# Attention queries stored column by column in eight interleaved blocks, and a dense prefetch that begins four passes later

## What is computed

```python
# attention: batch 2, heads 8, seq 768, head_dim 64, 8 memory rows, chunks of 32
for c in range(nc):
    q_c = q[:, :, c_start:c_end]
    k_full = np.concatenate([mem_k, k[:, :, l_start:r_end]], axis=2)
    v_full = np.concatenate([mem_v, v[:, :, l_start:r_end]], axis=2)
    scores = scale * np.matmul(q_c, k_full.transpose(0, 1, 3, 2))
    a = np.exp(scores - np.max(scores, axis=-1, keepdims=True))
    a = a / (np.sum(a, axis=-1, keepdims=True) + 1e-09)
    out[:, :, c_start:c_end] = np.matmul(a, v_full)
# dense: 1536 tokens, 512 -> 2048 -> 512
h = x @ w_in
y = (h * (1.0 / (1.0 + np.exp(-1.702 * h)))) @ w_out
# then: one of 8 experts per token, 512 -> 1024 -> 512, times its gate
```

## Time and profile before

| | us |
|---|---|
| median of 3 runs | 571.86 |
| lowest and highest | 567.55, 575.18 |
| the profiled execution, its own time | 572.34 |
| its span, first to last instruction | 570.6 |
| attention: first score matmul to end of the last values | 7.7 to 82.9 |
| mean granted TensorE clock | 0.97 of 2.4 GHz |

### The profile page before, as it was taken

The page is one execution under the profiler, slowest core; times in us unless marked ns, Lnnn a source line. Parts: engine busy times, 40 slices in busy tenths (PEclk is TensorE's granted clock), DMA queues, the critical chain, the costliest instruction groups (busy, mean ns, idle before and its releaser), DMA issues.

```text
span 570.6 us, 8633 instructions
## 1 busy us (share of the span) xinstructions
PE 534.4 (94%) x3228; PEld 453.2 (79%) x3228; DVE 286.4 (50%) x541; ACT 222.7 (39%) x374; POOL 174.8 (31%) x207
## 2 busy tenths in 40 slices
PE   7988889999999999999999999789999989999792
PEld 7878778888888878888887887679989878788582
DVE  4985666444233342213445545515445467756950
ACT  1443474334232221213334344114546366755520
POOL 2764530000000002000000300202576488999642
PEclk9996799999999999999999999898999999999997
DMA  7999919920000001001222532244947287766000
GB/s 206 254 267 242 213 48 350 286 68 0 1 0 2 1 1 71 4 0 38 74 75 75 181 114 75 93 130 150 337 141 278 83 312 248 263 237 223 22 24 30
DMA packets 33130, 74.39 MB, mean 130 GB/s; under 512 B 5423, under 2 KB 12335, under 8 KB 33072
## 3 DMA queue, kind: packets, MB, share of 16 engines
q1 hardware_dynamic: 28800, 66.97, 38.4%
q0 software_dynamic: 3840, 6.32, 3.1%
q10 hardware_dynamic: 432, 0.33, 0.2%
HBM read 60.97 MB, written 18.91 MB: 140 GB/s over the span
## 4 chain that ended last, share of the span: by engine, by line
PE 83%; DMA 5%; DVE 4%; issue 4%; POOL 1%; SPq 1%; ACT 1%; DVEq 0%; POOLq 0%
PE bank L1076 10%; PE bank L1078 10%; PE bank L1077 10%; PE bank L1120 8%; PE bank L1121 8%; PE bank L1122 8%; PE bank L1089 5%; DMA tile_in<-attention_tiles 5%; PE bank L1040 3%; PE bank L1293 3%; PE bank L1291 3%; PE bank L1292 3%; PE bank L1091 2%; PE bank L1191 2%; PE bank L1289 2%
## 5 line engine op out<-in xcount | busy, mean ns | idle before, releaser
L323 POOL TENSOR_TENSOR w_lo<-raw,w_hi 128x256 fp32r<-128x256 f32 x100 | 83.2, 867 | 51.8 <-ACT w_hi L307 51.7
L482 POOL DMA_INDIRECT dispatched_rows<-rows,slot_idx x12 | 11.9, 994 | 281.4 <-issue 147.8
L769 DVE SCALAR_TENSOR_TENSOR g<-g,bank 128x512 f32<-128x512 f32 x48 | 33.0, 688 | 112.6 <-ACT g L558 112.0
L307 ACT ACTIVATE w_hi<-raw 128x1024 fp32r<-128x1024 f32 x80 | 82.8, 1052 | 0.4 <-DMA raw<-expert_units 0.3
L558 ACT ACTIVATE g<-bank 128x512 f32<-128x512 f32 x48 | 28.8, 600 | 134.7 <-PE bank L1078 134.7
L323 DVE TENSOR_TENSOR w_lo<-raw,w_hi 128x1024 fp32r<-128x1024 f32 x55 | 75.4, 1371 | 8.3 <-ACT w_hi L307 8.0
L1120 PE MATMUL bank<-w_hi,g_hi 128*128 128x512 f32 x192 | 76.0, 396 | 1.5 <-issue 1.5
L1076 PE MATMUL bank<-x_hi,w_hi 128*128 128x512 f32 x192 | 76.7, 399 | 0.0
L1121 PE MATMUL bank<-w_lo,g_hi 128*128 128x512 f32 x192 | 75.8, 395 | 0.0
L1122 PE MATMUL bank<-w_hi,g_lo 128*128 128x512 f32 x192 | 75.8, 395 | 0.0
L1078 PE MATMUL bank<-x_hi,w_lo 128*128 128x512 f32 x192 | 75.7, 394 | 0.0
(11 more groups left out here) (119 smaller groups left out, 963.1 us busy)
## 6 DMA issues: line engine op xcount, KB each, us to landing
raw<-expert_units SPq DMA_DIRECT2D x64, 512.0 KB, 4.4
raw<-dense_units SPq DMA_DIRECT2D x16, 512.0 KB, 10.4
dispatched_rows<-empty SPq DMA_DIRECT2D x24, 257.0 KB, 12.6
slot_rows<-dispatched_rows SPq DMA_DIRECT2D x24, 257.0 KB
tile_in<-attention_tiles SPq DMA_DIRECT2D x12, 384.0 KB, 7.7
tile_in<-attention_tiles SPq DMA_DIRECT2D x12, 336.0 KB, 7.0
tile_in<-attention_tiles SPq DMA_DIRECT2D x12, 160.0 KB, 5.6
tile_in<-attention_tiles SPq DMA_DIRECT2D x12, 128.0 KB, 6.0
```

The costliest lines, as they stand in the source:

```text
L307: act.activation(w_hi[u % RING][:, :], raw[u % RING][:, :], ACT.Copy).then_inc(s_whi, 1)
L323: last = engine.tensor_tensor(w_lo[u % RING][:, part], raw[u % RING][:, part], w_hi[u % RING][:, part].bitcast(F32), ALU.subtract)
L769: dve.scalar_tensor_tensor(g32[i % 2][:, :], g32[i % 2][:, :], 1.0, h_bank[i % 2][:, :], ALU.add, ALU.mult).then_inc(s_g, 1)
```

## The change

Three things. First, the queries of a tile: the eight blocks are interleaved, so that column m of block x stands at column 8 m + x. The upper 64 partitions have their 64 x 8 query columns first and the zeros behind, the lower ones the reverse. A DMA row is now one run of 2048 bytes, the two query DMAs are 64 partitions by 512 columns each, together 256 KB where it was 288 KB, and the stationary matrix of block x is read with a stride of 8 columns, which is 32 bytes (`blocks[:, :, x]`). Second, both windows now have the same order of halves, so the values matmuls read the same side of the transposed probabilities in each. Third, `EARLY_FROM` is 9. The host lays the input out to match.

```diff
--- before.py
+++ after.py
@@ -42,10 +42,9 @@
     MAX_GROUPS = [GROUPS] + [[(0, NBL)]] * (B * S // P - 1)
     max_done = lambda t, g: sum(len(x) for x in MAX_GROUPS[:t]) + g + 1
     SCALE = 1.0 / D ** 0.5
-    Q_RUNS = 2 * NP + 1
-    QK = Q_RUNS * P + NP * SPAN
+    QK = NBL * P + NP * SPAN
     ATT = QK + WINDOWS * DM
-    Q_IN = (NP + 1) * P
+    Q_IN = NBL * HALF
     NSLOT = 3
     TB = 4
@@ -59,7 +58,7 @@
     UNITS = U0 + E * UE
     RING = U0
     EARLY = 8
-    EARLY_FROM = 5
+    EARLY_FROM = 9
     AHEAD = 4
     SLT = CAP // P
     SLOTS = E * CAP
@@ -291,14 +290,12 @@
             return (s_H, STEPS + EFT * e + 2 * r + 2) if r < UE // 2 else \
                 (s_Y, STEPS + EFT * e + 2 * (r - UE // 2) + 2)
-        def query_runs(n, half, odd):
-
-
-
-
-            runs = NP if odd else NP + 1
-            part = tile_in[n][half * D:(half + 1) * D, odd * P:odd * P + runs * 2 * P]
-            return part.rearrange("p (c x) -> p c x", x=2 * P)[:, :, 0:P]
+        def queries(n, half, place):
+
+
+
+
+            return tile_in[n][half * D:(half + 1) * D, place * Q_IN:(place + 1) * Q_IN]
         def split_hi(act, u):
             act.wait_ge(s_raw[u % RING], 16 * (u // RING + 1))
@@ -377,10 +374,9 @@
 
                 for half in range(2):
-                    there = attn_in[t, half * D:(half + 1) * D, 0:(NP + 1 - half) * P]
-                    sp.dma_start(query_runs(n, half, half), there.rearrange("p (c x) -> p c x", x=P))\
+                    sp.dma_start(queries(n, half, half), attn_in[t, half * D:(half + 1) * D, 0:Q_IN])\
                       .then_inc(s_qk[n], 16)
-                sp.dma_start(tile_in[n][:, Q_RUNS * P:QK], attn_in[t, :, Q_IN:Q_IN + NP * SPAN])\
+                sp.dma_start(tile_in[n][:, NBL * P:QK], attn_in[t, :, Q_IN:Q_IN + NP * SPAN])\
                   .then_inc(s_qk[n], 16)
             def load_values(t):
@@ -776,7 +772,7 @@
             for n in range(NSLOT):
                 for half in range(2):
-                    dve.memset(query_runs(n, half, 1 - half), 0.0).then_inc(s_zero_q, 1)
+                    dve.memset(queries(n, half, 1 - half), 0.0).then_inc(s_zero_q, 1)
             for t in range(-3, NT + 1):
                 if 0 <= t + 1 < NT - 1:
                     inverse(t + 1)
@@ -1035,10 +1031,11 @@
                 for g, (x0, x1) in enumerate(GROUPS):
                     if t >= 2:
                         pe.wait_ge(s_mask, NG * (t - 2) + g + 1)
+                    blocks = tile_in[n][:, 0:NBL * P].rearrange("p (m x) -> p m x", x=NBL)
                     for x in range(x0, x1):
-                        q0, k0 = HALF + x * P, Q_RUNS * P + x // WINDOWS * SPAN + x % WINDOWS * (HALF + M)
+                        k0 = NBL * P + x // WINDOWS * SPAN + x % WINDOWS * (HALF + M)
                         last = pe.matmul(score_bank[t % 2][g][:, (x - x0) * KEYS:(x - x0 + 1) * KEYS],
-                                         tile_in[n][:, q0:q0 + P], tile_in[n][:, k0:k0 + KEYS],
+                                         blocks[:, :, x], tile_in[n][:, k0:k0 + KEYS],
                                          start=True, stop=True)
                     last.then_inc(s_score, 1)
@@ -1063,8 +1060,7 @@
                         pe.wait_ge(s_pTa, NG * t + x // BPG + 1)
                     for half in range(2):
                         v0 = QK + w * DM + (2 * c + half) * D
-
-                        side = (half + w) % 2 * HALF
+                        side = half * HALF
                         last = pe.matmul(xT_bank[t % 2][half * D:(half + 1) * D, x * HALF:(x + 1) * HALF],
                                          tile_in[n][0:KEYS, v0:v0 + D],
                                          probT[t % 2][0:KEYS, x, side:side + HALF], start=True, stop=True)
@@ -1405,7 +1401,7 @@
     T, NT, TPB, KT = B * S, B * S // P, S // P, DM // P
     half = P // 2
     keys, span = half + LEFT + RIGHT + M, P + LEFT + RIGHT + 2 * M
-    q_in = (H // 2 + 1) * P
+    q_in = H * half
     f32 = np.float32
 
@@ -1413,8 +1409,9 @@
     for t in range(NT):
         b, s0 = t // TPB, t % TPB * P
         qt = q[b, :, s0:s0 + P].transpose(0, 2, 1)
-        attn[t, 0:D, half:half + H // 2 * P] = qt[0::2].transpose(1, 0, 2).reshape(D, -1)
-        attn[t, D:P, 0:H // 2 * P] = qt[1::2].transpose(1, 0, 2).reshape(D, -1)
+        for a in range(2):
+            blocks = qt[a::2].reshape(H // 2, D, 2, half).transpose(1, 3, 0, 2)
+            attn[t, a * D:(a + 1) * D, 0:q_in] = blocks.reshape(D, q_in)
         lo, hi = max(0, s0 - LEFT), min(S, s0 + P + RIGHT)
         kw = np.zeros((H, span, D), f32)
         vw = np.zeros((H, span, D), f32)
```

## The result

The changed kernel takes 584.02 us (median of 4 runs, 579.98 to 585.19) beside 572.09 for the one before (4 runs). The ratio is 1.020, with an interval of 1.012 to 1.029. So it is slower beyond the noise, though the interval does not tell whether by more than 2%. I had forecast 2.4% faster and a range of 553 to 579. The profiled execution takes 584.39 us, its span is 582.7.

What follows compares the result with a forecast made beforehand. Passes 3 to 8 were taken as bound by DMA, through the 512 KB unit in each turn. Terms -15.4 + 0.5 + 1.0 + 0.8 - 0.6 + 0 = -13.7 us from 572.34 gave 558.6, stated as 558.5; range 553 to 579.

Steps and rivals of the forecast that it cites:

- The strided weight load: Score matmuls' stationary loads with a stride of 8 words: taken as 0 us, at worst +1.86 us per tile if halved.
- Rival 1: The stride doubles the score load, TensorE bounds passes 0 to 8: +5.6 us, about 578; chance 0.21.
- start and first scores: Before pass 0: first three tiles' scores +4 us under the doubled load, earlier key issue -0.6 us.
- The prefetch: Passes 3 to 8, units moved four turns later: 23.1 us in place of 38.46, -15.4 us, no clock loss.
- rival 2: DMA stays the bound in part at 245 GB/s, passes 3 to 8 take 30.9 us: -7.5, near 565; chance 0.15.
- Does the DMA keep up?: Tile inputs in passes 3 to 8: 280 GB/s, 3.6 us per tile; 0 to +1.4 us, taken as +0.5.
- The two units in the way: Queries of tiles 10 and 11 behind one dense unit each: 0 to +4.7 us, taken as +1.0.
- The units in time: Dense units fetched later still land before ScalarE and the first dense steps want them: cost 0.
- the values: Values matmuls reading a different half of the tile in four of eight blocks: same count and shapes, 0.
- the tail: Pass 9, with VectorE and GpSimd late for pass 10 after a short pass 8: 4.35 us from 3.53, +0.8.
- Faster by over 2%: Chance that the whole time falls under 560.4 us: 0.50; slower by more, over 583.3, had 0.06.

Runs made afterwards that it cites:

- experiment 3: The changed kernel with the prefetch put back (EARLY_FROM = 5), so the strided load alone; 585.02 us, ratio 1.024 to the kernel before.
- experiment 5: The changed kernel with the stride for each tile's first four blocks only, neighbouring columns for the last four; 565.58 us, ratio 0.991 to the kernel before.
- experiment 2: The changed kernel with the stationary matrix read from neighbouring columns, its DMAs and prefetch kept; 560.49 us, ratio 0.980 to the kernel before.
- experiment 8: experiment 2 with one query DMA over 128 partitions in place of two of 64, same bytes; 552.11 us, ratio 0.972 to the kernel before.
- experiment 1: The kernel before with only the prefetch moved (EARLY_FROM = 9), neighbouring columns as before; 561.21 us, ratio 0.981.
- Experiment 7: The kernel before with the prefetch later still: EARLY_FROM = 11 took 556.95 us, ratio 0.975; EARLY_FROM = 10 took 558.12, ratio 0.977.

## Why the prediction was wrong

**The strided weight load** is the step that failed. I put the term at 0; it measured 2.0 us in each pass at the full clock (3.87 us for a tile's scores in place of 1.86), and 17.3 us by the start of pass 11, the lower clock included. I took 0 because an expert's rows show 128 neighbouring words read in 0.06 us, half of the 0.116 that the score load takes, and called this twofold slack. The slack is real for neighbouring words only. With each word on a line of its own 128 of them need 0.24 us, four times the 0.06, whatever the clock. So halving the best rate was the wrong reading of that row: the best rate is lost by a factor of four, as it would be if a read took one word where it could take four. The row is also of another kind of load: the expert's weights are rounded float32 (`fp32r`), the queries plain float32, and no run loads both with one stride. The Trainium skill (SBUF — State Buffer, Door 1: The DMA port swizzle) speaks of lines of 16 bytes and of two hits per line for the full rate; the runs agree, with 0.122 us at two words per line and 0.238 at one. With its lines the row would have given the right bound: 32 lines in 0.06 us are at most 1.9 ns each, 128 lines 0.24 us, an estimate. Its sentence that a stride of 4 fp32 is free the runs do not bear out.

**Rival 1** had the right mechanism, and put the time at 578 with a chance of 0.21. By its own terms: passes 0 to 2 +5.6 forecast, +6.7 measured; start and first scores +4.0 - 0.6 forecast, +2.7 measured, since the strided load hardly suffers from the low clock (48 first matmuls in 11.5 us, 0.240 each, where they took 8.3); passes 3 to 8 -4.2 forecast, +1.5 measured. The last is the gap, and most of it is the clock, which the rival left out. Six passes of 5.87 us would be 35.2, near its 34.3; they took 40.0. It was down in part of that stretch (mean 0.78) with TensorE never idle. In experiment 3 and with the stride of 16 bytes it was down in the same way (mean 0.75 from 27.2 to 81.5 us, and 0.82 from 27.5 to 80.6), again without idle time, while it held at 1.00 in experiment 5, where half of the loads are fast. My sentence that TensorE "never idles long, so I count no clock loss" took a row without idle time as enough for the full clock. That the waiting for weights is what lowers the clock is argued, not shown by a run that changes nothing else.

**The prefetch.** The step was right in kind and too large. Without the stride, in experiment 2, passes 3 to 8 take 60.68 - 29.67 = 31.0 us, -7.5 where my terms for them gave -15.4 + 0.5 + 1.0 = -13.9. That is rival 2 nearly to the number: it put them at 30.9 us, with 12.3 for passes 3 to 5 and 18.6 for 6 to 8, and 13.5 and 17.5 were measured. I gave it 0.15. So it is partly luck that experiment 2 ends at 560.5, near my 558.5: by the start of pass 11 only 6.3 of my 13.7 us are there, and the rest of the gain lies behind the logits, where I had said that nothing changes.

**Does the DMA keep up?** Mis-sized. I took 280 GB/s and 3.6 us per tile; it was 233 GB/s and 13.5 / 3 = 4.5 us in passes 3 to 5 of experiment 2, +0.65 per pass where my upper end was +0.23. I had put the rate down to the length of the rows; experiment 8 shows that the two query transfers of 64 partitions held it down.

**The two units in the way.** Forecast +1.0 of 0 to +4.7. In experiment 1 passes 7 and 8 take 62.17 - 48.30 = 13.9 us, 6.2 over two of 3.85: 2.5 us of wait, and most of the rest the low clock after it, which the term left out. Experiment 7 regains 4 us by moving the units. One count ahead of the prediction is wrong as well: with `EARLY_FROM` = 5 not four but six units have queries behind them (units 0 to 5, ahead of tiles 6 to 11). The sums don't use the four, since they take all of passes 3 to 8 as bound by the DMA.

**The units in time, the values, the tail** held in the changed kernel: no wait of ScalarE for units 0 to 3, values at the old pace at the full clock, passes 9 and 10 as before. The tail's +0.8 didn't come there, where VectorE has passes of 5.9 us to keep up in. It came in experiments 1 and 2: pass 9 takes 66.53 - 62.17 = 4.36 and 65.03 - 60.68 = 4.35 us, as forecast.

**Faster by over 2%** had 0.50, slower 0.06: that was too sure for an operation that no row of the trace shows. The 0.50 also counted a fifth of rival 2, whose own range began above the bound of 560.4.

## What to carry to other kernels

Keep the stationary operand's columns within 8 bytes of one another: for 4-byte words a stride of 2 is free here, a stride of 4 doubles the time from one score matmul to the next, from 0.116 to 0.238 us. When a layout for longer DMA rows costs a strided read, weigh both sides: here the rows brought 3 us where the DMA was the bound, the stride cost some 23. Look first at whether one transfer can reach all 128 partitions in place of two that reach 64 each; here that was worth 4 to 8 us of the whole time, and the block-diagonal zeros could be dropped with no loss that shows, by two small matmuls in opposite corners. Compare two kernels stage by stage too: a gain in the whole time may lie where the edit changed nothing.

## What the runs showed of the hardware

- A score matmul with a weight load of 128 fp32 columns takes 0.24 us at either clock level when the columns are 32 bytes apart, and 0.238 at 16 bytes, while one with neighbouring columns takes 0.116 at 2.4 GHz and about twice as much at 1.2: the scores at 44.71 of the kernel before, nearly all at the low level, take 3.73 us.
- A TensorE that shows no idle time can still be granted 1.2 GHz for part of it: mean clock 0.78 over 49.4 us of unbroken work, and whole tiles of scores at 0.50.
- Two DMAs of 64 partitions with 128 KB each in a tile's mixture: 233 GB/s, and 239 with dense units between; one of 128 partitions with 256 KB: 305 GB/s, at the same row length of 2 KB.
